# Attention, routing and two MLPs in one kernel: per-head score banks, outputs scaled on GpSimd, half of the token rows kept in SBUF

## The chip, the cores and the metric

One core of a Trainium2 chip runs the whole kernel: TensorE (PE), VectorE (DVE), ScalarE (ACT), GpSimd (POOL) and the DMA queues of SyncE (SP) and of GpSimd. The metric is the device time of one execution in microseconds, as the median of several runs. All inputs and outputs are float32 in HBM.

## The reference

Three stages follow each other; the output of one is the input of the next.

```python
# attention: q, k, v of shape (4, 8, 576, 64); heads 0-3 plain, heads 4-7 dilated
scores = q @ k.T / 8
rel = pos[:, None] - pos[None, :]
mask_plain = (rel >= 0) & (rel < 32)
mask_dil = (rel >= 0) & (rel < 128) & (rel % 4 == 0)
attn = softmax(where(mask, scores, -1e9)) ; x = attn @ v     # rows of 8 * 64 = 512
# mixture of experts on the 2304 token rows: x (2304, 512), 8 experts, w1 (8, 512, 1024), w2 (8, 1024, 512)
xn = x / (norm(x) + 1e-6) ; en = expert_emb / (norm(expert_emb) + 1e-6)
logits = xn @ en.T / tau ; expert = argmax(logits) ; gate = softmax(logits)[expert]
x = gate * (relu(x @ w1[expert]) @ w2[expert])
# last MLP: w_in (512, 2048), w_out (2048, 512)
h = x @ w_in ; out = (h * cos(h)) @ w_out
```

## The kernel before

Every engine has a program written out by hand, and all order comes from semaphores; nothing is scheduled by a tool.

**Attention.** A loop runs over the batch (b = 0 to 3). In it there are 12 steps: 4 pairs of heads, and for each pair 3 steps of two query tiles of 96 rows. Pairs 0 and 1 are plain heads, 2 and 3 dilated ones (their keys and queries are permuted into four strands, so that both kinds have a window of 32 + 96 keys per query tile). The text calls the three steps of a pair a, b and c. A step goes through these stages:

- M, L560: a bf16 matmul with the identity writes the additive mask into the score bank, 96x512, and S, L564: two matmuls add the scores of two tiles for both heads. The queries of both heads lie one below the other in `qT` (128 partitions), and `kT` has a copy for each head whose other 64 partitions are zero; so one matmul of 256 columns makes both heads' scores. Float32 matmuls show up as two records each.
- row maximum (DVE, L1156) and subtraction (DVE, L1159), then E, the exponential (ACT, L855).
- T, L573: four transposes of the probabilities into a bank, and P, L861: ACT copies them to SBUF.
- V, L585: four matmuls with the values, which have a column of ones for the denominator. `normalise` (DVE, L1179 to L1183) adds 1e-9, takes the reciprocal and multiplies, from PSUM into `osb`.
- In step b the next pair is prepared: Q, L548: six transposes of queries into banks 0 and 1; `q_out` (ACT, L845) copies them out half by half; K, L548: six transposes of keys into the same two banks, each half once `q_out` has freed it; `k_out` copies them to `kT`, the first half on ACT (L850), the second on DVE (L298), in two copies of 64 partitions each. M of the next step a waits for both halves.

PE's order in a step s is: M and S of s; Q if it is a step b; T of s-1; V of s-2; K if it is a step b. ACT's order is: `q_out` if it is a step b; E of s; P of s-1; `k_out` if it is a step b. DVE's is: maximum and subtraction of s; `normalise` of s-2; its `k_out`.

After the last step of a pair GpSimd issues the DMA of `osb` to the DRAM tensor `x_rows` (L492 once for a plain pair, L496 four times for a dilated one, whose permutation it undoes). When batch b-1 has been stored, SP reads its 576 rows back into `xtok` (L350), and ACT takes the six sums of squares in steps 6 to 11 of batch b (L868). In batch 0 PE also transposes the expert embedding (`experts`, L601).

**Routing.** For G = 0 to 11: transposes of two token tiles (L654), copies by ACT (L917) and DVE, logits (L638). For the last batch the sums of squares lie here. Then come 24 small transposes, the argmax on DVE, the inverse norms on GpSimd (14 linked operations, L278 to L285), the counts and places of the rows, a gather of the rows by expert (L516), and the expert blocks of 352 rows.

**Last MLP.** A hardware loop over m = 0 to 2 (768 rows each) with 32 units in its body, all float32 products made as three passes (L687 to L689), and the cosine chain between PE, ACT (L1025, L1037, L1040) and DVE (L1421 to L1438), which ends in `hid` (L1431). Units that differ by m stand under hardware `If`s.

## Time and profile before

| | us |
|---|---|
| median of 3 runs | 878.92 (878.09 to 881.27) |
| the profiled execution's own time | 879.44 |
| its span, first to last instruction | 877.5 |
| attention loop | about 12.5 to 142.6 |
| routing up to the first expert matmul | 142.6 to 194.6 |
| experts, then last MLP | 194.6 to 866 |

Busy time of an engine is the time in which it had an instruction running. Matmul records overlap, so the distance from one start to the next tells what a matmul costs, not its length. In the timeline a row is: start in us, duration, engine, source line, operation, output <- inputs, shapes, and in brackets the idle time before it with what ended it.

### The profile page before, as it was taken

The numbers are of one execution on the slowest core, as the hardware profiler recorded it, in microseconds if no ns is written. First come the engines' busy times: TensorE is split into PE (matmuls) and PEld (weight loads), VectorE is DVE, ScalarE is ACT, GpSimd is POOL, SyncE is SP. The second block draws the span as 40 slices with busy tenths as digits, with TensorE's granted clock in tenths as the row PEclk, the third lists the DMA queues.
The fourth block names the chain that finished last, engine by engine and source line by source line (L and its number), as shares of the span: only waits on it lengthen the run. The fifth ranks groups of instructions, "written<-read, shape, count | busy, mean of one in ns | idle before, by whom it ended". The sixth has DMA issues, their size and how long they took to land.

```text
span 877.5 us, 15798 instructions
## 1 busy us (share of the span) xinstructions
PE 823.3 (94%) x4902; PEld 745.4 (85%) x4902; DVE 607.6 (69%) x1169; ACT 481.4 (55%) x919; POOL 75.6 (9%) x134
## 2 busy tenths in 40 slices
PE   5999999749999999999989999999999999999993
PEld 3787876439999999999988999988999988999992
DVE  6888886575555566455567777778777788777762
ACT  3557765315545545444456666676656676656651
POOL 4022112141001000000000000001000002000002
PEclk9999999959999999999999999999999999999998
DMA  6498986234444443444242122123212214121001
GB/s 138 93 221 181 193 198 184 70 109 156 129 165 163 144 129 119 139 144 144 73 145 73 49 73 71 51 63 130 72 49 71 72 48 145 48 72 59 14 0 72
DMA packets 114911, 93.67 MB, mean 107 GB/s; under 512 B 65816, under 2 KB 94488, under 8 KB 114848
## 3 DMA queue, kind: packets, MB, share of 16 engines
q1 hardware_dynamic: 109920, 78.81, 31.1%
q0 software_dynamic: 4928, 14.16, 4.9%
q8 instruction: 23, 0.38, 0.2%
q14 instruction: 40, 0.33, 0.1%
HBM read 83.51 MB, written 9.44 MB: 106 GB/s over the span
## 4 chain that ended last, share of the span: by engine, by line
PE 78%; DVE 7%; DMA 5%; issue 4%; ACT 3%; POOL 1%; DVEq 0%; ACTq 0%; POOLq 0%; SPq 0%
PE bank L687 23%; PE bank L689 23%; PE bank L688 23%; DMA xtok<-x_rows 3%; PE bank L585 2%; PE bank L564 2%; PE bank L638 2%; PE bank L729 1%; PE bank L573 1%; DMA x_rows<-osb 1%; PE bank L654 1%; PE bank L548 1%; ACT yh L1010 1%; DMA dn_raw<-in_moe_w_out_dram 1%; DVE row_max L1156 1%
## 5 line engine op out<-in xcount | busy, mean ns | idle before, releaser
L687 PE MATMUL bank<-yh,up_l 128*128 128x384 f32 x384 | 129.7, 338 | 2.4 <-DVE yl L1409 2.4
L689 PE MATMUL bank<-yh,up_h 128*128 128x384 f32 x384 | 130.1, 339 | 0.0
L688 PE MATMUL bank<-yl,up_h 128*128 128x384 f32 x384 | 129.4, 337 | 0.0
L687 PE MATMUL bank<-dn_h,hid 128*128 128x512 f32 x288 | 113.0, 392 | 4.5 <-DVE hid L1431 4.2
L689 PE MATMUL bank<-dn_h,hid 128*128 128x512 f32 x288 | 113.9, 395 | 0.0
L688 PE MATMUL bank<-dn_l,hid 128*128 128x512 f32 x288 | 113.7, 395 | 0.0
L1219 DVE TENSOR_TENSOR dn_l<-dn_raw,dn_h 128x512 fp32r<-128x512 f32 (+1 forms) x80 | 71.9, 900 | 53.3 <-ACT dn_h L905 53.3
L1025 ACT ACTIVATE work<-bank 128x384 f32<-128x384 f32 x96 | 47.2, 491 | 81.4 <-PE bank L689 78.4
L687 PE MATMUL bank<-xh,up_l 128*128 128x352 f32 x256 | 85.2, 333 | 1.7 <-DVE xl L1351 1.4
L1037 ACT ACTIVATE work<-work 128x384 f32<-128x384 f32 x96 | 50.4, 525 | 66.0 <-DVE work L1426 66.0
L1421 DVE TENSOR_SCALAR work<-work 128x384 f32<-128x384 f32 x96 | 34.5, 360 | 75.3 <-ACT work L1025 75.3
L905 ACT ACTIVATE dn_h<-dn_raw 128x512 fp32r<-128x512 f32 (+1 forms) x80 | 63.7, 798 | 37.6 <-PE bank L689 37.6
L687 PE MATMUL bank<-hid,dn_l 128*128 128x352 f32 x256 | 83.0, 324 | 0.8 <-issue 0.8
L689 PE MATMUL bank<-xh,up_h 128*128 128x352 f32 x256 | 83.6, 326 | 0.0
L688 PE MATMUL bank<-xl,up_h 128*128 128x352 f32 x256 | 83.3, 325 | 0.0
L688 PE MATMUL bank<-hid,dn_h 128*128 128x352 f32 x256 | 83.0, 324 | 0.0
L689 PE MATMUL bank<-hid,dn_h 128*128 128x352 f32 x256 | 82.6, 323 | 0.0
L1219 DVE TENSOR_TENSOR up_l<-up_raw,up_h 128x512 fp32r<-128x512 f32 (+1 forms) x80 | 71.9, 899 | 11.1 <-ACT up_h L905 10.5
L687 PEld LDWEIGHTS bank<-yh,up_l 128*128 128x128 f32 x384 | 72.4, 189 | 6.8 <-DVE yl L1409 2.7
L971 ACT ACTIVATE hid<-bank 128x352 fp32r<-128x352 f32 x64 | 29.7, 464 | 84.9 <-PE bank L689 84.5
L688 PEld LDWEIGHTS bank<-yl,up_h 128*128 128x128 f32 x384 | 72.4, 188 | 4.0
L689 PEld LDWEIGHTS bank<-yh,up_h 128*128 128x128 f32 x384 | 72.3, 188 | 0.0
(194 smaller groups left out, 1659.1 us busy)
## 6 DMA issues: line engine op xcount, KB each, us to landing
up_raw<-in_moe_w_dram SPq DMA_DIRECT2D x32, 512.0 KB, 3.5
dn_raw<-in_moe_w_dram SPq DMA_DIRECT2D x32, 512.0 KB, 3.4
up_raw<-in_moe_w_in_dram SPq DMA_DIRECT2D x24, 512.0 KB, 3.2
dn_raw<-in_moe_w_out_dram SPq DMA_DIRECT2D x24, 512.0 KB, 3.4
qn<-in_q_dram SPq DMA_DIRECT2D x32, 144.0 KB, 2.8
kn<-in_k_dram SPq DMA_DIRECT2D x32, 144.0 KB, 3.3
xtok<-x_rows SPq DMA_DIRECT2D x4, 1152.0 KB, 7.5
x_rows<-osb POOLq DMA_DIRECT2D x8, 288.0 KB, 3.9
```

The lines of the kernel that those rows point to most:

```text
L564: last = mm(o[:QT, i * 256:(i + 1) * 256].rearrange("p (h c) -> p h c", h=2), qT[p % 2][:, t * QT:(t + 1) * QT], kT[p % 2][:, :, t * QT:t ...
L585: last = mm(bank[6 + s % 2][:QT, i * VN:(i + 1) * VN], probsT[s % 2][:, i * QT:(i + 1) * QT], vw[p % 2][:, 2 * u + i // 2, i % 2, :], star ...
L638: last = mm(bank[4 + G % 2][:E, 0:2 * QT], embT[:, d, :], xT[G % 2][:, d, :], start=d == 0, stop=d == DT - 1)
L687: mm(o, w[1], x[0], start=first, stop=False, skip_group_check=True)
L688: mm(o, w[0], x[1], start=False, stop=False, skip_group_check=True)
L689: return mm(o, w[0], x[0], start=False, stop=last, skip_group_check=True)
L905: A(hi[s][:, rows, :], raw[s][:, rows, :], ACT.Copy).then_inc(w[f"{which}_hi"], 1)
L971: A(hid[:, f % 4, 0, 0:TB], bank[4 + f % 4][:, 0:TB], ACT.Relu).then_inc(ex_h_hi, 1)
L1025: A(turns, bank[6 + i % 2][:, 0:HR], ACT.Copy, scale=1 / (2 * PI), bias=ROUND).then_inc(turns_ready, 1)
L1037: A(folded, red2, ACT.Abs).then_inc(folded_ready, 1)
L1219: ins = tt(lo[s][:, rows, :], raw[s][:, rows, :], hi[s][:, rows, :], ALU.subtract)
L1421: ts(whole, turns, ROUND, None, ALU.subtract).then_inc(whole_ready, 1)
```

## The change

- **Scores.** `kT` becomes one tensor of 128 partitions without the zero halves. Each head gets a PSUM bank of its own (`score[i][:, h, :]`, two buffers, banks 2 to 5). The mask is half as wide and is added twice (96x256 each); the scores become four matmuls of 64 partitions and 128 columns. `k_out` is one copy, not two, for each half. The transposed probabilities now have one bank (6) and the outputs one bank (7), where each had two.
- **Outputs.** A new ACT operation `outputs_raw` (R) copies outputs and denominators, 96x260, from bank 7 to `raw`. DVE keeps only the add and the reciprocal (`inverse`, at lag 3). GpSimd multiplies, for plain heads into `xtok`, for dilated heads into `osb`.
- **ACT's order** in a step s is now `q_out` (step b), E of s, R of s-2, P of s (was s-1), `k_out` (step b).
- **Rows.** Plain heads are stored to `x_rows` from `xtok`, and SP reads back only the dilated half of the columns.
- **Squares.** None in the attention loop; 18 on ACT and 6 on DVE in the routing loop.
- **Small things.** `experts` comes after attention; the wait for the inverse norms and the two operations behind it move to just before the last `in_lane` comparison; the last MLP is written out by Python instead of run in hardware loops with `If`s.

```diff
-        bank = [... psum_tensor(f"bank{i}", [P, 512], F32)) for i in range(8)]
+        score = [... psum_tensor(f"score{i}", [P, 2, 512], F32)) for i in range(2)]
-                mm(o[:QT, :], ident_bf[:], mask[...], start=True, stop=False)
+                for h in range(2):
+                    mm(score[s % 2][:QT, h, 0:2 * KW], ident_bf[:], mask[:, p // 2, 2 * u:2 * u + 2, :], start=True, stop=False)
                 for i in range(2):
                     t = 2 * u + i
-                    last = mm(o[:QT, i * 256:(i + 1) * 256], qT[p % 2][:, t * QT:(t + 1) * QT],
-                              kT[p % 2][:, :, t * QT:t * QT + KW], start=False, stop=True)
+                    for h in range(2):
+                        rows = slice(h * D, (h + 1) * D)
+                        last = mm(score[s % 2][:QT, h, i * KW:(i + 1) * KW], qT[p % 2][rows, t * QT:(t + 1) * QT],
+                                  kT[p % 2][rows, t * QT:t * QT + KW], start=False, stop=True)
...
+            def outputs_raw(b, s):
+                act.wait_ge(pv_done, b * STEPS + (s + 7))
+                act.wait_ge(norm_done, b * STEPS + (s + 3))
+                A(raw[s % 2][:], bank[7][:QT, 0:4 * VN]...[:, :, 0:D + 1], ACT.Copy).then_inc(pv_out, 1)
...
                     exps(b, s)
-                    if s >= 1:
-                        probsT_out(b, s - 1)
+                    if s >= 2:
+                        outputs_raw(b, s - 2)
+                    probsT_out(b, s)
                     if s % 3 == 1:
                         next_pair(b, s, k_out)
-                    if s in SQUARE_STEPS:
-                        before_this(act, b, lambda: squares(b, SQUARE_STEPS.index(s)))
...
+                pool.wait_ge(inv_done, b * STEPS + (s + 4))
+                g.tensor_tensor(o, raw[s % 2][:, :, 0:D]..., inv[:, s % 2, :]..., ALU.mult).then_inc(norm_done, 1)
...
-                sp.dma_start(xtok[:, bass.ds(last * NT, NT), :], x_rows[bass.ds(last * S, S), :]...)
+                sp.dma_start(xtok[:, bass.ds(last * NT, NT), DM // 2:], x_rows[bass.ds(last * S, S), DM // 2:]...)
...
-            with pe.Fori(0, NM) as m:
+            for m in range(NM):
```

## Rows read from the trace of the kernel before

**Rows 1.** The page: busy time, share and instructions of each engine

```profile
PE 823.3 (94%) x4902; PEld 745.4 (85%) x4902; DVE 607.6 (69%) x1169; ACT 481.4 (55%) x919; POOL 75.6 (9%) x134
```

**Rows 2.** Timeline, one pair of batch 1, from M of step b to the next

```profile
79.68 0.38 PE L560 MATMUL bank<-mask,ident_bf 96*96 96x512 bf16 x1
...
79.90 1.03 PE L564 MATMUL bank<-kT,qT 128*96 128x256 f32 x4
...
80.76 0.66 PE L548 MATMUL bank<-ident,qn 96*128 96x96 f32 x6
...
81.26 0.49 PE L573 MATMUL bank<-ident,probs 96*128 96x96 f32 x4
...
82.25 0.66 PE L548 MATMUL bank<-ident,kn 96*128 96x96 f32 x6
...
82.74 0.38 PE L560 MATMUL bank<-mask,ident_bf 96*96 96x512 bf16 x1
...
83.02 0.47 ACT L861 ACTIVATE probsT<-bank 128x384 f32<-128x384 f32 x1
...
83.39 0.81 ACT L850 ACTIVATE kT<-bank 64x288 f32<-64x288 f32 x2
...
84.81 0.38 PE L560 MATMUL bank<-mask,ident_bf 96*96 96x512 bf16 x1
...
85.58 0.63 ACT L855 ACTIVATE probs<-shifted 96x512 f32<-96x512 f32 x1 [1.38 <-DVE shifted L1159]
...
86.26 0.55 PE L573 MATMUL bank<-ident,probs 96*128 96x96 f32 x4 [0.20 <-ACT probs L855]
...
87.51 0.38 PE L560 MATMUL bank<-mask,ident_bf 96*96 96x512 bf16 x1
```

**Rows 3.** Timeline, batch 1, step 7: `q_out` late behind a square

```profile
66.14 0.68 ACT L845 ACTIVATE qT<-bank 128x288 f32<-128x288 f32 x2
...
66.58 0.77 PE L548 MATMUL bank<-ident,kn 96*128 96x96 f32 x6 [0.38 <-ACT qT L845]
```

**Rows 4.** Timeline, routing loop: transposes and ACT's copy of the first four

```profile
145.68 0.88 PE L654 MATMUL bank<-ident,xtok 96*128 96x96 f32 x8
...
146.27 0.49 ACT L917 ACTIVATE xT<-bank 128x384 f32<-128x384 f32 x1 [1.93 <-PE bank L654]
```

**Rows 5.** Timeline, batch 0: transposes of 8 partitions between full ones

```profile
23.93 1.03 PE L564 MATMUL bank<-kT,qT 128*96 128x256 f32 x4
...
24.89 0.41 PE L601 MATMUL bank<-ident,emb_sq 8*128 8x8 f32 x4
...
25.23 0.71 PE L548 MATMUL bank<-ident,qn 96*128 96x96 f32 x6
```

**Rows 6.** Timeline: M of step 1 of batch 0, and of the last step

```profile
14.63 0.63 PE L560 MATMUL bank<-mask,ident_bf 96*96 96x512 bf16 x1
...
137.16 0.38 PE L560 MATMUL bank<-mask,ident_bf 96*96 96x512 bf16 x1
```

**Rows 7.** GpSimd's groups by form: busy us, mean ns of one, idle before

```profile
L496 POOL DMA_DIRECT2D x_rows<-osb x32 | 18.1, 566 | 50.2 <-DVE osb L1183 47.6
...
L281 POOL TENSOR_TENSOR root_f<-root_f,ssq 96x24 f32<-96x24 f32 x3 | 0.7, 233 | 0.2
...
L281 POOL TENSOR_TENSOR emb_n<-emb_n 8x1 f32<-8x1 f32 x3 | 0.6, 185 | 0.2
```

**Rows 8.** Timeline, start: the masks, and the first M

```profile
8.61 2.78 DVE L1130 CAST mask<-band 96x256 bf16<-96x256 f32 x12
...
12.48 0.66 PE L560 MATMUL bank<-mask,ident_bf 96*96 96x512 bf16 x1 [2.58 <-DVE kT L298]
```

**Rows 9.** Timeline: end of attention, first transposes of the routing loop

```profile
142.66 1.49 PE L654 MATMUL bank<-ident,xtok 96*128 96x96 f32 x16
```

**Rows 10.** Who waited for whom, PE: us in total, times, longest

```profile
PE bank L687 <- DVE hid L1431: 4.2, 7, 1.0
```

**Rows 11.** Timeline, last MLP: ACT's first operation after the loop wraps

```profile
591.40 0.49 ACT L1025 ACTIVATE work<-bank 128x384 f32<-128x384 f32 x1 [1.45 <-issue]
```

More of the change, by code:

```diff
@@ L51, in fused_kernel @@
     QK_IN, PLAIN_IN, DIL_IN = 16 * 4, 16 * 2 * 3, 16 * 2 * 4
-    STORES = 16 * 5
-    SQUARE_STEPS = (6, 7, 8, 9, 10, 11)
+    STORES = 16 * 4
+    DVE_SQUARES = tuple(range(3, RT, 4))
+    ACT_SQUARES = tuple(t for t in range(RT) if t not in DVE_SQUARES)
     ROW_BANKS = (5, 6, 7, 4)
@@ L71, in sem @@
             return ctx.enter_context(nc.semaphore(name))
-        bank = [ctx.enter_context(nc.psum_tensor(f"bank{i}", [P, 512], F32)) for i in range(8)]
+        bank = [ctx.enter_context(nc.psum_tensor(f"bank{i}", [P, 512], F32)) for i in range(2)]
+        score = [ctx.enter_context(nc.psum_tensor(f"score{i}", [P, 2, 512], F32)) for i in range(2)]
+        bank += [score[i][:, h, :] for i in range(2) for h in range(2)]
+        bank += [ctx.enter_context(nc.psum_tensor(f"bank{i}", [P, 512], F32)) for i in range(6, 8)]
         ident = sb("ident", [P, P])
@@ L142, in fused_kernel @@
         qT = [sb2(f"qT{i}", [P, S]) for i in range(2)]
-        kT = [sb2(f"kT{i}", [P, 2, WINDOW + S]) for i in range(2)]
+        kT = [sb2(f"kT{i}", [P, WINDOW + S]) for i in range(2)]
         shifted = [sb2(f"shifted{i}", [QT, 4 * KW]) for i in range(2)]
@@ L147, in fused_kernel @@
         osb = [sb2(f"osb{i}", [QT, NT, 2, D]) for i in range(2)]
+        raw = [sb2(f"raw{i}", [QT, 4, D + 1]) for i in range(2)]
         row_max = sb2("row_max", [QT, 2, 4])
@@ L270, in before_this @@
         def before_this(eng, i, work):
+            if isinstance(i, int):
+                if i > 0:
+                    work()
+                return
             with eng.If(i > 0):
@@ L287, in half_out @@
         def half_out(copy, p, half):
-            for h in range(2):
-                rows = slice(h * D, (h + 1) * D)
-                o = kT[p % 2][rows, h, WINDOW:WINDOW + S]
-                i = bank[half][rows, 0:3 * QT]
-                if p % PAIRS < PAIRS // 2:
-                    o = o[:, half * 3 * QT:(half + 1) * 3 * QT]
-                else:
-                    o = o.rearrange("p (r i) -> p r i", r=DIL)[:, :, half * SEG // 2:(half + 1) * SEG // 2]
-                    i = i.rearrange("p (i r) -> p r i", r=DIL)
-                last = copy(o, i)
+            o = kT[p % 2][:, WINDOW:WINDOW + S]
+            i = bank[half][:, 0:3 * QT]
+            if p % PAIRS < PAIRS // 2:
+                o = o[:, half * 3 * QT:(half + 1) * 3 * QT]
+            else:
+                o = o.rearrange("p (r i) -> p r i", r=DIL)[:, :, half * SEG // 2:(half + 1) * SEG // 2]
+                i = i.rearrange("p (i r) -> p r i", r=DIL)
+            last = copy(o, i)
             last.then_inc(tr_out[half], 1)
@@ L628, in _ @@
             times_v(B, -1)
+            experts()
             def logits(G):
@@ L818, in _ @@
                     else:
-                        with pe.If(m > 0):
+                        if m > 0:
                             mlp_up(m, i)
@@ L921, in _ @@
                     expert_dn_hi(0, 0)
-                if G >= (B - 1) * NT // 2:
-                    for t in range(2):
-                        squares(B, 2 * G - (B - 1) * NT + t)
+                for t in range(2 * G, 2 * G + 2):
+                    if t in ACT_SQUARES:
+                        squares(t)
             act.wait_ge(shifted_ready, 1)
@@ L1071, in _ @@
             act.sem_inc(carrier, 1)
-            with act.Fori(0, NM) as m:
+            for m in range(NM):
                 for i in range(2 * FT2):
@@ L1129, in _ @@
                 for t, w in enumerate(which):
-                    last = cp(mask[:, kind, t, :, :], band[:, w:w + 1, :].broadcast_to([QT, 2, P]))
+                    last = cp(mask[:, kind, t, :], band[:, w, :])
             last.then_inc(init_done, 1)
@@ L1207, in _, with square_sums @@
                             emb_rows()
-                    if s == 4:
-                        with dve.If(b < 1):
-                            experts_out()
-            normalise(B, -2)
-            normalise(B, -1)
+            for s in (-3, -2, -1):
+                inverse(B, s)
+            experts_out()
+            def square_sums(t):
+                dve.wait_ge(x_in, 16 * (t // NT + 1))
+                dve.wait_ge(ssq_done_d, DVE_SQUARES.index(t) + 1)
+                V.tensor_tensor_reduce(sq_junk_d[:], xtok[:, t, :], xtok[:, t, :], 1.0, 0.0, ALU.mult, ALU.add,
+                                       ssq[:, t:t + 1]).then_inc(ssq_done_d, 1)
             def weights_lo(w, which, raw, hi, lo, hi_count, parts=1, part=0, s=0):
@@ L1461, in _ @@
             dve.sem_inc(carrier, 1)
-            with dve.Fori(0, NM) as m:
+            for m in range(NM):
                 for i in range(2 * FT2):
```

151 lines of the change are left out of this document (79 added, 72 removed).

## The prediction

> **What bounds the kernel now.** I read the page first: PE is busy 94% of the span and DVE 69% [rows 1]. A busy PE says little by itself, so I went on to the timeline of the one place that the change rebuilds, the attention loop, and followed M, the first matmul of a step, from start to start. A pair of heads takes 87.51 - 79.68 = 7.83 us: b to c 3.06, c to a 2.07, a to b 2.70 [rows 2]. What PE must issue in it: the mask 0.22 (79.68 to 79.90), the scores 0.86 (79.90 to 80.76), T and V 0.99 (81.26 to 82.25), so 2.07 in each step, and Q 0.50 and K 0.49 once: 7.2 us. Step c is exactly its 2.07; step b is 2.07 + 0.99. Only step a has a gap, 0.6 us, in which T waits for E (86.26 behind 85.58). So the loop is bound by PE's issue with a small wait in each pair. DVE is near: two 96x512 passes and `normalise` fill it almost wholly, and that is what makes E late in step a.
>
> From M of the second step of batch 0 to M of the last step there are 15 pairs and a step, 137.16 - 14.63 = 122.5 us [rows 6]. 15 x 7.83 + 2.07 is 119.5, so 3.0 us are extras: the embedding work in batch 0, and squares that hold up `q_out`, as where K waits 0.38 us for it [rows 3]. In the last MLP PE waits 4.2 us in all for `hid`, seven times [rows 10]; three of these, of 1 us each (about 2.9 together), stand behind a loop entry or wrap, where ACT sits 1.45 us with nothing to wait for but its own issue [rows 11].
>
> **Scores, the price X.** X is what PE spends from the first score matmul to the next operation, 0.86 now. Four matmuls of 128 columns have the same columns as two of 256; a gain comes only if the two heads, on partitions 0 to 63 and 64 to 127, run side by side. No row shows that. Each float32 matmul is two records, in the order A, A, B, B for heads A and B; if starts stay in order, one record of A and one of B overlap at each change of head, and eight records of 0.107 (half of 0.215, 0.86 / 4) take five slots, 0.54. Weight loads could be next: V and T, eight and four small weight loads with their matmuls, keep a pace of 0.08 each (0.99 / 12) [rows 2], so eight take 0.66. Bounds: 0.54 (perfect in order) and 0.86 (no overlap); I take 0.60.
>
> To this comes a second price. 
>
> The Trainium skill's page "TensorEngine Tiling (Array Packing)", Key Properties, says that changing the tiling mode drains TensorE; these rows agree, with 0.24 us for the two changes. Its page "TensorE: Matmul & The Clock Gate", Part 3, has matmuls of different row groups starting about 4 ns apart and finishing in order; by that the scores alone would be 0.54 us.
>
> **The handoffs.** ACT's new order moves P of step s forward into step s, ahead of the next step's `q_out` and ahead of `k_out`. But P needs T, and PE issues T of step s only after M and S, and in step b after Q, of s+1. What queues behind that wait on ACT: in step b `q_out`, which K needs; then `k_out`, which M of the next step a needs. The pieces: T to P 0.59 (145.68 to 146.27, also four transposes) [rows 4]; P to the next ACT operation 0.37 (83.02 to 83.39); one half of `q_out` 0.34, and its start to the transposes that it frees 0.44 [rows 3].
> - b to c: mask 0.22, X, Q 0.50, T to P 0.59, P 0.37, first half 0.34, handoff 0.44, last three transposes of K 0.25: 2.71 + X. PE alone would need 2.20 + X.
> - c to a: 0.22, X, T to P 0.59, P 0.37, `k_out` and its handoff 0.44: 1.62 + X. PE alone 1.21 + X.
> - a to b: 0.22, X, T and V 0.99: 1.21 + X. E is not late here: E came 2.84 us after M with X of 0.86, T 0.68 after E, so T at 2.66 + X after M of c against 1.84 + 2X; the two meet at X of 0.82.
> A pair: 5.54 + 3X = 8.09, against 7.83. The loop: 15 x 8.09 + 2.06 + 0.5 of embedding work left = 123.9, against 122.5: **+1.4 us**. The squares and the early `experts` (2.5 of the 3.0) are already out of it. The pair breaks even at X = 0.76.
>
> **Outputs.** DVE loses a multiply of about 0.4 a step and one of two key copies; it stops being near the bound, worth nothing while the handoffs rule. R on ACT, 96x260 from PSUM, lies between a half of `q_out` (128x288, 0.34) and P (0.47): 0.37. It falls into the time in which ACT waits for T: hidden. GpSimd's multiply isn't in the trace: two-input operations take 0.233 for 24 elements and 0.185 for one, 2.1 ns an element, so 0.185 + 0.54 = 0.7 for 256; bounds 0.23 and twice the slope, 1.3 [rows 7]. It is due when R reuses its buffer two steps later. The hard place is behind a dilated pair: multiply, four DMA issues of 0.57 with gaps (2.6), multiply; from the reciprocal to that R there are about 5.2 us, so a multiply may take up to 1.3. Hidden. For plain pairs one DMA issue: more room. Reading back half the rows shortens a transfer that nobody waits for any more, as the squares have left the loop; the last one is due only at G = 9, some 20 us after attention ends: nothing.
>
> **Start.** Twelve mask copies of 2.78 us [rows 8] become half as wide (some 0.8 less, as part of each is fixed), and one key copy goes (0.45): **-1.3**.
>
> **End of attention.** From the last M to the first L654: 142.66 - 137.16 = 5.50 [rows 6, 9]. After: T at 2.66 + X = 3.5; V of 46 (0.33 on), read 0.9 later, R 0.4; V of 47 had to wait for that bank; again 0.9 and 0.4; `experts` 0.3: 6.8. **+1.3**. The routing loop is 2.2 us of PE in each turn; ACT has 0.49 and at most two squares of 0.8 in it, so the moved squares are hidden. In the argmax part DVE no longer waits for the inverse norms (0.4), but does their two operations of 0.35 ahead of the last comparison: **+0.3**.
>
> **Last MLP.** Without wraps ACT's 1.45 us of issue are gone, and with them the three waits of PE: **-2.8**, bounds -3.2 and 0.
>
> Sum: +1.4 - 1.3 + 1.3 + 0.3 - 2.8 = -1.1 us. The profiled execution took 879.44 (span 877.5), so 878.3; the median of the runs is 0.5 lower: 878.92 - 1.1 = **877.8 us**. Over X from 0.79 to 0.91 (0.54 or 0.66 with the 0.25) it is 875.1 to 880.5.
>
> **Rivals.**
> - Overlap without a price for the switches: X of 0.54 to 0.66. Then E rules from c on and a pair takes 2.71 + X + 2.66 + X + 0.99 = 6.36 + 2X, 7.44 to 7.68: 867.8 to 871.4. For it: two banks let both heads write at once. Against: [rows 5].
> - No overlap: the heads run one after the other and the switches are paid, X = 1.11, a pair 8.87: 15 x 0.78 + 0.3 more, **889.8**, slower. It decides from X of about 0.97 on. For it: no row shows two matmuls side by side.
> - The handoffs don't bind, PE's issue does: 4.62 + 3X = 7.17, 863.5. Against: the order of the queues as written.
> - GpSimd late: a multiply over 1.3 us, or DMA issues slower beside it, holds R, then V, in the eight dilated pairs; 0.5 us each gives 882.
>
> **How the numbers follow.** The forecast's mechanism 0.42, and its times lie mostly within 0.5% (4.4 us, about what this measurement can tell from no change); cheap switches 0.20; no overlap 0.15; handoffs hidden 0.07; GpSimd late 0.08; other 0.08. Faster: 0.20 + 0.07 + a tenth from the forecast's lower edge and the rest, 0.37. Slower: 0.15 + 0.05 + 0.05, 0.25. Same 0.38. The range takes in the first rival and just the second: 866 to 890; the forecast's own is 873 to 882.
>
> **What would show it.** M to M in a pair of 3.56, 2.47 and 2.06; K's first half behind `q_out`, with PE idle there about 0.5 us; M of step a behind `k_out`, idle 0.4; score records of the two heads overlapping, and 0.1 us before and after them; no PE wait for GpSimd; no waits of 1 us for `hid` at multiples of 126 us. The prediction is wrong if X is off (0.1 us in X is 4.6 us of time), or if ACT takes `q_out` before P's wait matters.

## The result, and the profile after

The changed kernel takes 891.09 us (median of 6 runs, 885.18 to 898.25), the kernel before 878.50 beside it (6 runs, 876.82 to 881.27): a ratio of 1.0139 with a 95% interval of 1.0109 to 1.0169. It is **slower by 1.4%**. I had forecast 877.8 us, no change, with 866 to 890 as the range; the median lies just outside it. Its runs also spread over 13 us where those of before spread over 4.5. The profiled execution is the fastest of the six, 885.18 us with a span of 883.6, so only 6 of the 12.6 us can be read in it. The ratios further down stand against the kernel before as it ran beside each group of experiments (medians of 878.7 to 879.9 us), and leave out runs that lie more than 1.5% above the fastest of their kernel.

I read the page first. PE's share has fallen from 94% to 93%, but the span has grown [rows 1]:

```profile
PE 823.2 (93%) x5142; PEld 744.9 (84%) x5142; DVE 582.8 (66%) x1117; ACT 485.4 (55%) x939; POOL 105.3 (12%) x182
```

Then the timeline of one pair in batch 2, from M of step c (L595) over a and b to M of the next c; it answers to [rows 2].

```profile
87.65 0.38 PE L595 MATMUL score<-mask,ident_bf 96*96 96x256 bf16 x2
87.96 0.68 PE L601 MATMUL score<-kT,qT 64*96 64x128 f32 x8
88.57 0.55 PE L610 MATMUL bank<-ident,probs 96*128 96x96 f32 x4
...
90.00 0.42 PE L595 MATMUL score<-mask,ident_bf 96*96 96x256 bf16 x2 [0.22 <-ACT kT L883]
...
92.01 0.38 PE L595 MATMUL score<-mask,ident_bf 96*96 96x256 bf16 x2
...
94.86 0.77 PE L583 MATMUL bank<-ident,kn 96*128 96x96 f32 x6 [0.22 <-ACT qT L878]
95.47 0.38 PE L595 MATMUL score<-mask,ident_bf 96*96 96x256 bf16 x2
```

M to M is 2.35, 2.01 and 3.46: 7.82 us, against 7.83 before and 8.09 forecast. The two waits of the forecast stand there (K for `qT`, M of step a for `kT`). M to T takes 0.92 in step c; less the mask's old 0.22 this is X = 0.70, not 0.85.

So a warm pair, one at TensorE's full clock, costs what it did, and the loop is still longer: from the second M, 13.78, to the last, 142.71, it is 128.9 us against 122.5 [rows 6]. The start of the timeline shows the largest piece:

```profile
14.37 1.17 PE L601 MATMUL score<-kT,qT 64*96 64x128 f32 x8
...
18.29 1.22 PE L583 MATMUL bank<-ident,kn 96*128 96x96 f32 x6 [0.96 <-ACT qT L878]
19.30 0.63 PE L595 MATMUL score<-mask,ident_bf 96*96 96x256 bf16 x2
19.87 1.17 PE L601 MATMUL score<-kT,qT 64*96 64x128 f32 x8
...
22.90 0.63 PE L595 MATMUL score<-mask,ident_bf 96*96 96x256 bf16 x2
```

The eight score records take 1.17 us here and 0.68 in the pair above: TensorE runs at its lower level (1.2 GHz instead of 2.4) from the first M to about 30 us. Before, its records were short from 16.5 us on. That the stretch is one of low clock is read from these lengths. Four steps of 5.52, 3.60, 3.60 and 5.02 stand where warm ones would take 3.46, 2.35, 2.01 and 3.46: +6.5 us. The column of the granted clock doesn't show this stretch (it reads 1.00 there); the lengths are those of later stretches where it reads 0.50 (e17 below).

The two longest waits for values in the loop of this execution are of 1.14 and 1.20 us. Behind neither did the clock fall; the first:

```profile
81.19 0.87 PE L622 MATMUL bank<-vw,probsT 128*96 128x72 f32 x8 [1.14 <-DMA vw<-in_v_dram]
...
82.29 0.68 PE L601 MATMUL score<-kT,qT 64*96 64x128 f32 x8
```

The end of attention, POOL, ACT and PE, answers to [rows 9]:

```profile
146.96 2.59 POOL L529 DMA_DIRECT2D x_rows<-osb  x4 [0.73 <-POOL osb L509]
149.51 1.26 POOL L509 TENSOR_TENSOR osb<-raw,inv 96x256 f32<-96x256 f32 x2
...
150.29 0.38 ACT L899 ACTIVATE raw<-bank 96x260 f32<-96x260 f32 x1 [2.77 <-POOL osb L509]
...
150.82 0.56 PE L638 MATMUL bank<-ident,emb_sq 8*128 8x8 f32 x4 [2.28 <-ACT raw L899]
151.31 1.54 PE L688 MATMUL bank<-ident,xtok 96*128 96x96 f32 x8
```

The last R waits 2.77 us until GpSimd, which is issuing four stores, gets to the multiply that frees `raw`; PE waits 2.28 for it, and then makes eight transposes in 1.54 us where eight later ones take 0.88. The last MLP keeps three short waits for `hid` (its rows of PE's waits) where it had seven of up to 1.0 [rows 10]:

```profile
PE score L720 <- DVE hid L1458: 0.9, 2, 0.5
PE bank L720 <- DVE hid L1458: 0.6, 1, 0.6
```

The ledger of the two profiled executions, after minus before: start up to the second M -0.9; loop +6.4 (low clock +6.5, waits for transfers about +2.7, the extras of before -3.0); last M to the first L688 +3.1 (8.60 against 5.50); from there to the first expert matmul +2.3 (54.2 against 52.0); experts -0.6; last MLP, from its first matmul to the end of its last `hid`, -4.3 (405.7 against 410.0). Sum +6.0, the spans differ by 6.1.

### The profile page after: what moved, and what is told of

Read it like the earlier page. It is cut to its first block, busy times and chain, and to the rows that moved or that the text cites. A ratio compares the mean times of both kernels' runs of the same rounds, so it can differ in the third digit from the quotient of the medians.

```text
span 883.6 us, 15866 instructions
## 1 busy us (share of the span) xinstructions
PE 823.2 (93%) x5142; PEld 744.9 (84%) x5142; DVE 582.8 (66%) x1117; ACT 485.4 (55%) x939; POOL 105.3 (12%) x182
## 4 chain that ended last, share of the span: by engine, by line
PE 80%; DVE 6%; issue 4%; SPq 3%; DMA 3%; ACT 2%; POOL 1%; ACTq 0%; POOLq 0%; DVEq 0%
PE bank L720 14%; PE bank L722 14%; PE bank L721 14%; PE score L721 9%; PE score L720 9%; PE score L722 9%; SPq L353 3%; PE score L670 2%; PE score L601 2%; PE bank L583 1%; PE bank L622 1%; DMA vw<-in_v_dram 1%; PE bank L610 1%; DVE yl L1436 1%; DMA x_rows<-osb 1%
## 5 line engine op out<-in xcount | busy, mean ns | idle before, releaser
L562 POOL DMA_INDIRECT out_dram<-osb,id_now x18 | 18.9, 1048 | 565.2 <-ACT osb L1083 550.4
L720 PE MATMUL score<-dn_h,hid 128*128 128x512 f32 x192 | 75.1, 391 | 1.1 <-DVE hid L1458 0.9
L722 PE MATMUL score<-dn_h,hid 128*128 128x512 f32 x192 | 75.8, 395 | 0.0
L721 PE MATMUL score<-dn_l,hid 128*128 128x512 f32 x192 | 75.8, 395 | 0.0
L1465 DVE TENSOR_TENSOR work<-bank,work 128x384 f32<-128x384 f32 x96 | 53.5, 558 | 18.8 <-ACT work L1075 18.8
L941 ACT ACTIVATE up_h<-up_raw 128x512 fp32r<-128x512 f32 (+1 forms) x80 | 63.5, 795 | 2.3 <-issue 2.3
L1075 ACT ACTIVATE work<-work,half_pi 128x384 f32<-128x384 f32 x96 | 59.3, 618 | 3.1
L1453 DVE SCALAR_TENSOR_TENSOR work<-work 128x384 f32<-128x384 f32 x96 | 53.6, 558 | 3.3
L1450 DVE SCALAR_TENSOR_TENSOR work<-work,bank 128x384 f32<-128x384 f32 x96 | 53.2, 555 | 3.3
L1458 DVE TENSOR_TENSOR hid<-work,hid 128x384 fp32r<-128x384 f32 x96 | 52.9, 551 | 0.2 <-ACT hid L1066 0.2
```

What stands on the lines that cost most here:

```text
L720: mm(o, w[1], x[0], start=first, stop=False, skip_group_check=True)
L721: mm(o, w[0], x[1], start=False, stop=False, skip_group_check=True)
L722: return mm(o, w[0], x[0], start=False, stop=last, skip_group_check=True)
L941: A(hi[s][:, rows, :], raw[s][:, rows, :], ACT.Copy).then_inc(w[f"{which}_hi"], 1)
L1075: A(cosine, folded, ACT.Sin, scale=-1.0, bias=half_pi[:, 0:1]).then_inc(cosine_ready, 1)
L1450: stt(red1, whole, -TWO_PI_HI, h, ALU.mult, ALU.add).then_inc(red1_ready, 1)
```

## The experiments

Five edits come back in several kernels. Their texts, shortened (`...`, and the lines in brackets):

```diff
# fill: twelve useless matmuls ahead of the loop, 3 before Q, 3 before K, 6 before the first M
+            mm(bank[7][:, 0:P], ident[:], ident[:], start=True, stop=True, ...)
# tail: experts() writes bank[6] and waits pt_out; last outputs_raw and inverse move behind G = 0
+                pe.wait_ge(pt_out, B * STEPS + 4)
+                    last = tp(bank[6][:, d * E:(d + 1) * E], emb_sq[...], ident[:E, :E])
# order: ACT's queue in a step
                     exps(b, s)
                     outputs_raw(b, s - 2)
-                    (q_out stood ahead of exps in step b)
+                    if s % 3 == 0:
+                        next_pair(b, s, q_out)
+                    if s % 3 == 1:
+                        next_pair(b, s, k_out)
                     probsT_out(b, s)
# rows late: SP's read-back behind load_v of the last pair; rows mid: behind load_v of the third pair
# full rows: the score matmul takes qT[...][:, ...] and kT[...][:, ...], 128 partitions
```

**e1_after_again.** The changed kernel once more.

> The changed kernel unchanged, profiled a second time. Its first profile belonged to its fastest run (885.2 us); its six runs spread over 885 to 898, those of the kernel before over 877 to 881. Theory A (slow TensorE at the start): the score step's eight records take 1.17 us until about 30 us into the first profile and 0.68 after it, and where this stretch ends differs from run to run; then this profile, if its own time differs from 885, shows the same pace of 7.8 us a pair once warm and a slow stretch of another length: about 6.5 us lost if it ends at 30 us again, some 0.5 us more for each step that runs slow. Rival B (transfers): the pace of all pairs is unequal, waits for DMA at the values and the keys in every batch account for the difference, and the slow stretch ends at the same time.

889.06 us (5 runs, 886.13 to 892.37), ratio 1.0102 (1.0069 to 1.0135); the profile is of an 889.06 run. The slow start is the same. A second slow stretch lies in the loop, behind a wait for values:

```profile
82.25 0.87 PE L622 MATMUL bank<-vw,probsT 128*96 128x72 f32 x8 [1.07 <-DMA vw<-in_v_dram]
83.12 0.41 PE L595 MATMUL score<-mask,ident_bf 96*96 96x256 bf16 x2
83.47 0.98 PE L601 MATMUL score<-kT,qT 64*96 64x128 f32 x8
...
86.87 1.17 PE L601 MATMUL score<-kT,qT 64*96 64x128 f32 x8
```

and here the windows show it in the granted clock (the last three numbers are PEclk, DMA share and GB/s):

```profile
80.00:91.00 11.00, 9.92 (x73) 0.69 0.78 176
91.00:100.00 9.00, 8.56 (x94) 1.00 0.61 143
```

The pair from 79.70 took 3.42, 3.19 and 5.10, 11.7 us for 7.8: 3.9 us lost, of which 1.07 are the wait and 2.8 the low clock behind it. Both theories hold a part: a transfer comes late, and the low clock makes it dear. But the wait alone doesn't decide: at the same place of the first profile one of 1.14 us cost nothing more. The Trainium skill, page "TensorE: Matmul & The Clock Gate", section "HAM oscillation", describes matmul groups that lose the clock to DMA waits between them. The waits there are longer than this one; e1 agrees in that the clock fell behind a DMA wait, the first profile shows that after such a short wait it need not.

**e2_fill.** fill alone.

> The changed kernel with twelve 128x128 float32 matmuls of the identity into a bank that nothing reads, put in TensorE's three idle stretches before the attention loop (before the first Q, before the first K, before the first mask). Theory A: TensorE runs slow at the start because it is idle and narrow there; kept busy from about 4.5 us on, it is at full pace before or soon after the first mask, the first four steps take 11.4 us and not 17.7, so 5 to 7 us come off, and the spread of the runs shrinks to that of the kernel before: about 880 to 884. Rival B (waits for transfers in the loop): nothing of it changes, 0 to -1 us. Rival C (the handoffs among TensorE and ScalarE make the first steps long, whatever the pace of TensorE): 0 to -2 us.

883.90 us (10 runs, 881.09 to 896.65), 1.0053 (1.0029 to 1.0077): 5.2 less than e1. No score group at the start is longer than 0.68; from the second M the four steps take 4.52, 2.35, 2.39 and 3.46, 12.7 us for 17.7. The size was right, the spread was not: the profile, an execution of 893.47 us, has nine slow steps in the loop from 109 to 144 us, behind another wait for values, of 1.10 us. A slow start and slow stretches in the loop are two losses. That the spread is the low clock can be read from each run's mean granted clock over the whole execution: 881.45 and 882.27 us have 0.972 and 0.976, 888.84 has 0.961, 893.47 has 0.956, 896.65 has 0.951. The runs of the changed kernel itself don't follow it so well: 892.73 us has 0.962, but the two longest, 898.25 and 896.36, have 0.974 and 0.975, next to 0.977 for the fastest. A slow start isn't in that number; whether theirs was longer is not on record.

**e3_full_rows.** full rows alone; both heads' products are added, their separation is left out.

> The changed kernel with each of the four score matmuls over all 128 rows in place of one head's 64; this adds both heads' products together and so leaves out their separation; columns, banks, handoffs and all other work stay. The 64-row form measures 0.73 us from the first score to the next operation, with about 0.1 to 0.2 us for leaving and entering it. If full rows run one after the other, the score part takes 0.86 and its neighbours lose their gap: X of 0.86, a pair of 5.54 + 3 x 0.86 = 8.12 against 7.82, 15 pairs +4.5 us. Theory A adds: full rows keep TensorE's pace up as in the kernel before, so the slow stretch ends at about 16 us and not 30, -5 us: sum about -1 to 0, with a small spread of the runs. Rival (the width of the matmuls has nothing to do with the slow stretch): +4.5 us, and the spread stays.

884.18 us (6 runs, 883.82 to 885.54), 1.0050 (1.0030 to 1.0069). A pair takes 3.58 + 2.47 + 2.12 = 8.17 us, as forecast, so 5 us more than e1 in the loop, and the kernel is 4.9 us faster all the same. The start is warm at 18.9 us, no step in the loop is slow, and the runs lie within 1.7 us. But a slower pair also lets all values come in time (behind the start, no wait for a transfer of over 0.2 us in the loop), so this alone doesn't part the width from the waits.

**e4_before_mlp.** The kernel before with the last MLP's loop written out.

> The kernel before with the last MLP's loop written out, and nothing else of the change. Prediction: the three waits of 1 us each for hid at loop entry and wraps go: -2.8 us. From the profile of the changed kernel, where the MLP took 405.7 us against 410.0: -4.3 us. Rival: the written-out code costs instruction loading or the waits move elsewhere: 0 or slower.

875.83 us (10 runs, 873.95 to 876.67), 0.9959 (0.9948 to 0.9971): -3.4 us, between forecast and profile. Three waits for `hid`, 1.5 us in all, are left of 4.2.

**e5_tail.** tail alone.

> The changed kernel with only the end of attention untied: the transposes of the experts' embeddings go to the bank of the probability transposes, and ScalarE's last raw copy and VectorE's last reciprocal move behind the first copies of the routing loop; the bank of that last copy is waited for only where routing next writes it. In the changed kernel that last raw copy waits 2.77 us for GpSimd's multiply of two steps earlier, which sits behind four DMA issues of 2.59 us, and TensorE then runs at half its clock until about 156 us. Theory D (GpSimd's queue sets the end of attention): TensorE's 2.28 us of waiting go, and the slow stretch behind it (about 3 us) goes with it or shrinks: -2.3 to -5 us, 883 to 887. Rival: the wait only moves to the next bank or to the tokens that come in, 0 to -1 us. The spread of the runs, put down to lapses inside the loop, stays.

883.69 us (10 runs, 880.43 to 895.51), 1.0045 (1.0025 to 1.0064): 5.4 under e1. In the profile the last M to the first L688 is 143.99 to 150.74, 6.75 instead of 8.60, although a V there waits 1.27 us for values; the 2.28 us of waiting behind GpSimd's stores are gone. What the median shows beyond this 1.9 us can't be told from the spread. The spread stayed, as expected.

**e6_rows_late.** rows late alone.

> The changed kernel with the read-back of a batch's token rows moved in SyncE's queue from before the values of the third pair to behind those of the last pair. In the changed kernel this queue sits up to 3.4 us at the read-back, because the last dilated pair's stores are issued only at 91.9 us (84.0 before), and TensorE then waits 1.0 to 1.2 us for the last pair's values in two of the batches. In the second profile and in that of the filled start, the clock fell within two steps behind just such a wait (steps of 3.42 and 3.89 us), and each stretch of low clock cost 4 to 15 us. Theory B+A (the waits for transfers cost 1 us each and set off the lapses): -2.5 us from the waits, no lapses inside the loop, and runs that spread no more than 5 us: about 884 to 886, with the slow start still in. Rival (lapses come from the shape of the work alone, whatever the transfers do): -2.5 us at most, spread unchanged at 10 us or more.

898.80 us (4 runs, 897.08 to 901.69), 1.0219 (1.0186 to 1.0253). My expectation was wrong in sign. The read-back of 576 KB now stands right before the next batch's keys, PE waits 2.2 us for them at 89 us, and the step takes 7.03, then 3.60, 3.60 and 5.52 at low clock. A wait of 1.15 us for the next batch's keys, at 130 us, left the clock up. The start, too, stayed slow until 44 us in this execution.

**e7_order.** order alone.

> The changed kernel with two pieces of ScalarE's order swapped: q_out stands ahead of the probability copy P of the first step of a pair, and k_out ahead of P of the second; nothing else. Theory C (the handoffs of the new order cost what TensorE saves): a pair goes from 7.82 us to TensorE's own issue, 4.62 + 3 x 0.73 = 6.81, plus what the exponentials' chain still holds up, about 0.3: 7.1 us, 15 pairs -10.8 us; K no longer waits for qT, nor the mask for kT; with the idle time gone the slow stretch at the start should end earlier too. About 875 to 880. Rival (the exponentials bind, in the form of the prediction 6.36 + 2X = 7.82): a pair stays at 7.8 us and the time at 889. Second rival: GpSimd, with 2.6 us of DMA issues and three multiplies of 0.63 in a dilated pair, becomes the bound: the dilated pairs stay at 7.8, half of the gain.

887.95 us (4 runs, 884.84 to 899.13), 1.0137 (1.0067 to 1.0208). The pair did what was forecast, from its timeline (M of steps b, c, a and b):

```profile
87.85 0.38 PE L595 MATMUL score<-mask,ident_bf 96*96 96x256 bf16 x2
...
90.82 0.38 PE L595 MATMUL score<-mask,ident_bf 96*96 96x256 bf16 x2
...
92.79 0.38 PE L595 MATMUL score<-mask,ident_bf 96*96 96x256 bf16 x2
...
94.06 0.55 PE L610 MATMUL bank<-ident,probs 96*128 96x96 f32 x4 [0.28 <-ACT probs L888]
...
95.10 0.28 PE L595 MATMUL score<-mask,ident_bf 96*96 96x256 bf16 x1
```

2.97 + 1.97 + 2.31 = 7.25 us: neither K nor M waits for ACT, only T of step c by 0.28 for the exponentials. The time didn't follow. SP's queue shows why:

```profile
54.66 1.13 SPq L332 DMA_DIRECT2D kn<-in_k_dram  x2
59.24 0.33 SPq L361 DMA_DIRECT2D xtok<-x_rows  x1
59.81 5.93 SPq L353 DMA_DIRECT2D vw<-in_v_dram  x8
66.15 0.88 SPq L332 DMA_DIRECT2D qn<-in_q_dram  x2
```

From 55.8 to 59.24 it sits at the read-back, whose stores GpSimd issues only after its late multiplies; the eight loads of values behind it come late in both dilated pairs, PE waits 1.9 us, and the clock falls. Of this profile's waits for values, those of 1.89 and 1.54 us had slow score groups behind them (one and three), one of 1.49 had none. With a faster pair the transfers are the next thing to be late, and such a wait can be paid for several times.

**e8_all.** fill, tail, rows late and order.

> The changed kernel with all four edits: the filled start, the end of attention untied, the read-back late, and ScalarE's order swapped. If they add up: -5 (start), -2.5 (transfers), -3 (end), -10.8 (order), from 889: about 868, and runs that spread no more than those of the kernel before. If one common cause stands behind several of them (idle TensorE in the loop), less than the sum: 872. Rival: the exponentials or GpSimd bind: 878.

882.89 us (10 runs, 876.69 to 890.77), 1.0035 (1.0004 to 1.0066). Far from 868: three slow stretches, behind waits of 1.6 us for values and of 2.4 and 2.9 for keys; the loop from 13.02 to 144.21 is 131.2 us.

**e9_gp_rows_all.** fill, tail and order, and the read-back issued by GpSimd.

> The changed kernel with the filled start, the end of attention untied and ScalarE's order swapped, and the read-back of the token rows issued by GpSimd (ahead of the store of the next batch's second pair) in place of SyncE. With ScalarE's order swapped a pair measured 7.24 us, but SyncE sat 3.4 us at the read-back (55.8 to 59.24 us), TensorE then waited 1.9 us for the values of the last pair, and the clock fell. Theory: without the read-back in SyncE's queue these waits go (the queue needs 8.2 us for a dilated pair, 5.3 for a plain one, 27 of the 29 us of a batch, so a wait of some tenths may stay), no lapses follow, the loop takes 16 x 7.24 and some 2 to 3 us more, 118 to 120: 868 to 872, and a spread like that of the kernel before. Rival: SyncE's own issues bind (8.2 against 7.24 us): a wait of over 1 us for values stays once a batch, lapses stay, 877 to 883.

889.69 us (4 runs, 886.12 to 896.66), 1.0110 (1.0079 to 1.0141). The rival was right in kind, and too low: four waits for values, 10.3 us in all, the longest 3.2, and twelve slow score groups behind them.

**e10_full_all.** e8_all with full rows (the heads' separation is left out).

> The same kernel as e8_all (filled start, end untied, read-back at the batch's end in SyncE's queue, ScalarE's order swapped), with the score matmuls over all 128 rows (both heads' products are added: their separation is left out). It keeps the waits for transfers that e8_all had, 2.4 us for the keys at each batch's start and 1.6 us for values. e8_all had the clock low in three stretches behind such waits. Theory W (the half-width matmuls are what lets the clock fall, or stay low): the same waits, but the records at half speed are few, a step or less behind each wait; a pair of 7.24 + 3 x 0.12 = 7.6 us; about 16 x 7.6 + 3 x 2.4 + 2 = 131, and 876 to 879 with a small spread. Theory S (the wait alone does it): the clock falls behind each wait of over 1.5 us just as in e8_all and stays low for three to four steps: 885 to 890 with a wide spread.

877.34 us (10 runs, 874.00 to 880.55), 0.9977 (0.9958 to 0.9997). Its waits for keys stand at the same places but are shorter (1.78 and 1.83 us, where e8 had 2.43 and 2.92), and behind each only one score group is long (1.75 and 1.71 against 1.04), and the next is at full speed. The median is some 5.5 us below e8, though a warm pair is 0.4 slower.

**e11_gp_rows.** The changed kernel with only the read-back issued by GpSimd.

> The changed kernel with only the read-back of the token rows moved from SyncE's queue to GpSimd's, ahead of the store of the next batch's second pair. The move within SyncE's queue had made it worse, since the 576 KB read then stood right before the next batch's keys (a wait of 2.2 us, and lapses behind it). Here nothing stands behind it in SyncE's queue. Theory: the waits of 1.0 to 1.2 us for values go, and with them the lapses inside the loop: -2.5 us, with runs of 884 to 887 and the slow start still in. Rival: GpSimd's queue is now late with the multiplies, or the transfer itself delays the values whichever queue issued it: no gain, spread of 10 us as before.

895.84 us (4 runs, 891.14 to 898.18), 1.0179 (1.0137 to 1.0221). Wrong again: the waits for values grew, to 2.6 and 1.6 us in the loop. Which of the rival's two reasons it was isn't shown.

**e12_padded** and **e14_half_rows2.** Both: fill, tail, order, rows mid. e12 has the scores of the kernel before (keys beside zeros), in four matmuls of 128 rows; e14 those of the changed kernel. This is the comparison of the widths with both kernels complete; the second key copy goes with the wide form.

> The changed kernel with the filled start, the end untied, ScalarE's order swapped, SyncE's read-back behind the values of the third pair (where its stores have long landed, so that the queue does not sit there), and the scores of the kernel before: keys written twice beside zeros, each head's products over all 128 rows, four matmuls of 128 columns in the heads' own banks. In e10_full_all (full rows, both heads added) a pair took 7.60 us, one step behind each wait for transfers was slow, and three waits of 1.4 to 1.8 us with what followed cost about 9 us. Theory W (full-width work keeps or quickly regains the clock) and the queue: a pair of 7.6 us again, VectorE and ScalarE hide the second key copies (0.45 and 0.4 us), waits of 0.5 us or so per batch: last mask at about 131 us, 869 to 872, spread of 5 us. Rival: values of the last pair come late all the same, by 1 to 2 us per batch: 876. Second rival: the second key copies show, 0.3 us a pair: +5 on either.

> As e12_padded, but with the half-width score matmuls and single key copies of the changed kernel: the pair that tells the width of the matmuls apart with everything else alike and both kernels complete. A pair of 7.24 us where the clock is up. Theory W (half width lets the clock stay low after any wait): slow stretches of several steps at half speed (steps of 3.6, 3.6, 5.5) behind waits for transfers, a wide spread, 878 to 885, so slower than e12_padded although each warm pair is 0.36 us faster. Rival (it was only the waits that the read-back made): none or few slow steps, 865 to 868, faster than e12_padded by 5.

e12: 877.55 us (0.9984, 0.9964 to 1.0004; but for one outlier of 2883.46 its runs lie in 876.33 to 881.45). e14: 883.28 us (1.0043, 1.0006 to 1.0079; 878.73 to 896.82). The same place in both, step b of the last pair of batch 2, where the queries and keys of batch 3 come in behind the read-back; first e12, with a wait of 1.33 us:

```profile
104.98 0.71 PE L585 MATMUL bank<-ident,qn 96*128 96x96 f32 x6 [1.33 <-DMA kn<-in_k_dram]
...
107.23 1.04 PE L602 MATMUL score<-kT,qT 128*96 128x128 f32 x8
```

then e14, with 2.14 us:

```profile
108.58 1.22 PE L583 MATMUL bank<-ident,qn 96*128 96x96 f32 x6 [2.14 <-DMA kn<-in_k_dram]
...
112.99 1.17 PE L601 MATMUL score<-kT,qT 64*96 64x128 f32 x8
...
116.03 0.64 PE L595 MATMUL score<-mask,ident_bf 96*96 96x256 bf16 x2
```

and the windows of PE behind it, e12 and e14 (busy us and instructions, PEclk, DMA share, GB/s):

```profile
110.00:130.00 20.00, 19.70 (x209) 1.00 0.77 178
```

```profile
110.00:130.00 20.00, 19.73 (x143) 0.61 0.56 132
```

PE is as busy in both, but e14 gets through 143 instructions and e12 through 209. A warm pair is 7.24 us in e14 and 7.62 in e12; the loop from the second M is 132.7 us in e14 and 123.6 in e12. The wait in e14 is longer, probably since its loop runs ahead, so this place alone doesn't part width and wait; but e1 lost the clock for two steps to 1.07 us and e2 for nine to 1.10, and e10, full-width, lost it for one to 1.8. Nor is it this execution alone: the mean granted clock is 0.972 to 0.979 over the nine runs of e12, and in e14 it falls as the time grows, from 0.971 at 878.73 us over 0.962 at 883.91 to 0.952 at 890.70.

Width isn't the whole rule. At the start of routing the two change places: in e12 the transposes and logits of the first two turns run at low clock (0.50 from 146 to 150 us) and take 5.41 us, in e14 they take 3.01 at full clock. The waits just before are alike (0.63 and 0.56 us; 0.27, 0.47 and 0.56). e10 is like e12 there, e8 and e16 like e14.

**e13_before_best.** e4_before_mlp with fill, and all squares moved to the routing loop.

> The kernel before with the last MLP written out (875.8 us by itself), the twelve filler matmuls at the start, and all squares of the token rows taken out of the attention loop into the routing loop (all on ScalarE: two of 0.62 us beside one copy of 0.49 in a turn of 2.2 us). From the steps of before: two slow score steps at the start cost about 1.4 us, the squares hold up a step in three batches by 0.65, 0.45 and 0.33 us: 875.8 - 1.4 - 1.4 = 873. Rival: those steps were late because of the values' transfers, not of the squares, and routing gets longer by some ScalarE time: 875 to 876.

871.63 us (4 runs, 871.57 to 873.09), 0.9907 (0.9881 to 0.9934), **faster than both kernels**. The fill gave what was forecast (the first two steps to 17.02 and not 18.36 us), the squares almost nothing in the loop (118.7 us from there, against 118.9 in e4): the two steps of e4 that were late behind a square (3.68 and 3.71 us) are back at 3.07, but others are now late by values (1.4 us in two waits). So both forecasts held a part, and the sum came out better than either; where the rest came from wasn't looked for.

**e15_filled_loop**, **e16_filler_first**, **e17_short_filler.** e14 with a useless full-width matmul in every step. In e15 it stands between mask and scores in the mask's bank; token values and routing are then others (it seems that the mask of the first head no longer counts), so only its loop is read. In e16 it stands ahead of the mask, in e17 there too but with 32 columns for 128. The edit of e16:

```diff
                 pe.wait_ge(sub_done, b * STEPS + s + 1)
+                mm(score[s % 2][:, 0, 2 * KW:2 * KW + 128], ident[:], ident[:, 0:128], start=True, stop=True, ...)
                 for h in range(2):
```

> As e14_half_rows2, with one full 128x128 float32 matmul of the identity added to every step, into columns of the score bank that nothing reads: 0.21 us of useless work a step, 0.64 a pair, 10 us in all. Theory W: full-width work brings the clock back within a step or two behind a wait; a pair of 7.24 + 0.64 = 7.88, no long slow stretches, a small spread, 879 to 882; against e14 it costs less than its 10 us, or nothing. Rival: the clock doesn't depend on such a filler; slow stretches as in e14, and 10 us more than e14: 890.

> e15 with its filler matmul put ahead of the mask matmuls. In e15 it stood between mask and scores in the mask's bank and started an accumulation of its own, and the mask of the first head no longer counted: all later token values, and with them the routing, were others, so that only its loop can be read (12.07 to 137.13 us, no step at half speed, a pair of 7.70, against 12.22 to 146.13 in e14_half_rows2). Here the computation is whole. Theory W: the loop as in e15, 125 us, and the rest as in e12_padded or e14: 876 to 879 with a spread of 5 us, so 0.2 us of useless work in each step makes the kernel some 5 us faster than e14_half_rows2. Rival: the loop of e15 was quick because of its other values, or the mask's start flag; then slow stretches as in e14 and 890.

> e16 with the filler cut from 128 to 32 columns (still 128 rows by 128): a quarter of its work, some 0.1 us a step instead of 0.2, most of it the weight load. Theory W in its simple form (the share of full-width work brings the clock back): slow stretches shorter than in e14_half_rows2 (3 to 4 steps) but not gone, 877 to 883. If a single full-width instruction a step were enough, no slow steps, a pair of about 7.5, and 873 to 875. If it does nothing: as e14, 883 and a spread of 10 us or more, plus up to 4 us of its own.

e15: no slow step, a pair of 7.70, the loop 12.07 to 137.13; the time, 937.15 us, is that of another routing. e16: 878.90 us (10 runs, 875.79 to 885.00), 0.9994 (0.9974 to 1.0014): a pair of 7.77, no slow step in the loop, and 4.4 us **less** than e14, for 0.53 us more work in each pair. The intervals of the two just touch; the mean granted clock of its runs is 0.970 to 0.981. The same place of batch 2 shows a wait of 1.30 us and full speed behind it:

```profile
104.36 0.71 PE L583 MATMUL bank<-ident,qn 96*128 96x96 f32 x6 [1.30 <-DMA kn<-in_k_dram]
...
106.96 0.68 PE L602 MATMUL score<-kT,qT 64*96 64x128 f32 x8
```

(the first row, its M and its neighbours are at the lengths of a warm pair.) e17: 897.59 us (877.66 to 915.24 in four runs, too far apart for a ratio); the four runs with their mean granted clocks are 877.66 at 0.975, 891.23 at 0.957, 903.95 at 0.940 and 915.24 at 0.928. In its profile, of the run of 891.23, nine score groups in a row are slow, 75 to 111 us, after a wait of 1.7:

```profile
70.00:90.00 20.00, 18.76 (x118) 0.55 0.55 129
90.00:110.00 20.00, 20.00 (x125) 0.50 0.37 83
```

PE is busy for all of 20.00 us at half its clock. A quarter of the filler doesn't keep the clock up reliably: by the mean clocks it did in one run of four.

## Why the prediction was wrong

- **The step that failed** is the sum itself: "a pair: 5.54 + 3X", "the loop: 15 x 8.09 + ...". It gave +1.4 us for the loop, with every duration taken at full clock and nothing for a wait for transfers. The loop of the kernel before has one slow stretch, up to 16.5 us, and I priced nothing for it or for its return. In the best run the loop is +6.4: against the 123.9 us of the forecast, 6.5 of low clock at the start and about 2.7 of waiting for transfers come on top, and the faster pair (7.82 for 8.09) gives 4 back. e2 filled the start and took its 5 us off. The median run lies 6 us higher still; e1 shows a further slow stretch (2.8 us behind its wait), and how much of the 6 is such stretches isn't shown. e12 against e14 and e16 against e14 say that the half-width scores make them long. None of the rivals had this either.
- **The handoffs** were right in mechanism and place: M to M 3.46, 2.35, 2.01 for 3.56, 2.47, 2.06; e7 took them out and got 7.25 us. **X** was mis-sized: 0.70 for 0.85. The heads do overlap, S to T is 0.61, and 0.87 in e12 where each head takes all rows; the switch costs 0.09 ahead of the scores (M to S 0.31, 0.22 in e12) and at most what is in the 0.61 beyond 0.54 behind them, together 0.16, not 0.25. With X at 0.70 the sum of the handoffs would give 7.64 for a pair, 0.18 under what was measured, so the two errors partly cancelled. By the prediction's own condition the exponentials should have ruled step a at an X under 0.82; in the trace T of that step doesn't wait for them, M waits 0.22 for `kT`.
- **"GpSimd ... hidden"** was right in the loop (the multiply takes 0.61 to 0.63 for my 0.7) and wrong at its end. There V of the last step starts 1.4 us behind the one before it, not a step later, so its R is due at about 148.5, and four store issues of 2.59 us stand in front of the multiply that it waits for: my 6.8 us for the end became 8.60. e5 took the wait out.
- **"Reading back half the rows: nothing"** missed the queue. The stores of a batch's last pair are issued 9.9 us after the first M of the next batch (91.89 against 81.95) where it was 7.0 (83.98 against 76.98), SP sits at the read-back in front of the values, and PE waits 1.14 and 1.20 us for them. e6 and e11 moved the read-back alone and were slower than the changed kernel. With the other edits in, behind the last pair's values (e8, 882.89) and behind the third's (e14, 883.28) came out alike, and issued by GpSimd (e9, 889.69) worse; those edits with the read-back left in its place were not run.
- **Start** -0.4 for -1.3 up to the first M: the masks fell from 2.78 to 1.71 and a key copy went, but the copy of `band` ahead of them took 1.72 us for 0.73. In e11 it took 0.22 and the masks 3.04. So copy and masks together need 3.3 to 3.4 us where they needed 3.5, and halving the masks gained next to nothing. Why is open.
- **Routing** +2.3 for +0.3: its first transposes and logits run at low clock up to about 156 us (0.50 from 151 to 157). Its first two turns take 5.42 us for 3.02, and from there to the first expert matmul it is 48.8 for 49.0, so this stretch is the whole of it. In e8, e14 and e16 the two turns are back at 3.01.
- **Last MLP** -4.3 in the profile, -3.4 by itself (e4), for -2.8: right in mechanism (the waits for `hid` fell from 4.2 to 1.5 us), and a little beyond its bound of -3.2.

Left open: what in a half-width matmul keeps the clock down, why a wait of 1.07 us set it off and waits of 1.14 to 1.49 did not, why the full-width e12 lost it at the start of routing, and how much of the 6 us between the best run and the median is low clock.

## What to carry to other kernels

Before a change makes the matmuls narrower or the loop faster, look for the waits of 1 us that TensorE has or will have, and price them at both clocks: here a pair that was 0.6 us quicker (7.25 against 7.83) made the kernel no faster, since a wait could then cost nothing more, or 3 us (e1), or 18 (e17, nine steps in 41.4 us where warm ones take 22.9). When PE is 100% busy and gets through fewer instructions, compare the length of one instruction between stretches. Filling idle time ahead of a loop with useless matmuls is worth a try (5 us here in the changed kernel), and so is a wider form of the same product. When runs of one kernel spread, set each run's mean granted clock beside its time before explaining a single profile.

## What the runs showed of the hardware

- With half-width scores, half-speed score groups followed waits of 1.07 (e1), 1.10 (e2) and 1.54 us (e7), and none followed waits of 1.14 and 1.20 (first profile), 1.15 (e6) and 1.49 (e7). Behind every wait of over 1.54 us in the loop there were some. Such stretches were 1 to 9 groups long; with full-width scores, or a full-width filler of 128 columns, none or 1 (e10, e12, e16; waits up to 1.8 us).
- At the start the granted clock is shown as 1.00 while matmuls take 1.17 us for 0.68; later stretches with the same lengths show 0.50.
- A 0.2 us useless matmul per step lowered the time by 4.4 us (e16 against e14).
- Four float32 score matmuls on 64 rows, the two heads on different halves of the partitions and in different banks, took 0.61 us up to the next operation, the same on 128 rows 0.87 (e12); going from the mask's 96 rows to 64 cost 0.09 more than to 128.
- A matmul that starts an accumulation in other columns of a bank seems to end the one that was open there (e15 against e16); only the outcome was seen.
